# Attention, soft mixture of experts and a two-layer network on one core: ten ring slots, w_in and w_out loaded last, first token group in another order

## What is computed

```
attention:  q, k, v [4, 8, 576, 64]; scores = q k^T / 8 + bias by distance, causal window of 128, softmax, times v
x  = the heads side by side, 2304 tokens x 512
experts (soft mixture, 8 experts x 4 slots = 32 slots):
  logits = x @ phi;  d = softmax over tokens;  c = softmax over slots
  slot_input = d^T @ x                                   # 32 x 512
  slot_out[e] = relu(slot_input[e] @ w1[e]) @ w2[e]      # w1[e] 512 x 1024, w2[e] 1024 x 512
  y = c @ slot_out                                       # 2304 x 512
network:    h = relu(y @ w_in);  out = (h * h) @ w_out   # w_in 512 x 2048, w_out 2048 x 512
```

## Time and profile before

| | |
|---|---|
| median of three runs | 449.99 us (448.69 to 450.9) |
| the profiled execution | 451.01 us, span in the trace 449.4 us, mean granted clock of TensorE 0.973 |
| PE busy | 412.1 us, 92% of the span |
| DVE busy | 256.2 us, 57% |
| ACT busy | 208.4 us, 46% |
| last expert product ends | 215.40 us |
| first `project` starts | 230.86 us |
| share of PE in the chain that ended last | 78% |

### The profile page before, as it was taken

How to read it: one execution, slowest core, us unless ns; L and a number is a source line. 1 busy time by engine, 2 the same in 40 slices (tenths; PEclk the granted TensorE clock), 3 DMA queues, 4 the chain that set the end, 5 groups by cost and what they waited for, 6 DMA issues and landing times.

```text
span 449.4 us, 7858 instructions
## 1 busy us (share of the span) xinstructions
PE 412.1 (92%) x2851; PEld 312.3 (69%) x2851; DVE 256.2 (57%) x700; ACT 208.4 (46%) x541; POOL 71.7 (16%) x61
## 2 busy tenths in 40 slices
PE   4488999999989888966899999999999999999996
PEld 3376787878767544321368888888888888888884
DVE  3989989899872634210289745454444545454430
ACT  1456787877872311000197544434443444344420
POOL 2334556475660010000000000000000000000000
PEclk9979999999999989998599999999999999999999
DMA  5786999998743968999700100001010101010101
GB/s 135 170 233 177 231 265 237 255 259 202 188 112 131 402 254 300 413 388 387 291 0 1 47 2 16 30 1 47 2 47 2 47 0 47 0 47 0 48 0 47
DMA packets 73410, 61.35 MB, mean 137 GB/s; under 512 B 58784, under 2 KB 58784, under 8 KB 71328
## 3 DMA queue, kind: packets, MB, share of 16 engines
q1 hardware_dynamic: 73376, 60.89, 43.9%
HBM read 56.16 MB, written 4.72 MB: 135 GB/s over the span
## 4 chain that ended last, share of the span: by engine, by line
PE 78%; DVE 7%; ACT 5%; DMA 5%; SPq 3%; issue 1%; DVEq 0%
PE psum L1177 15%; PE psum L1175 15%; PE psum L1176 15%; ACT probs L752 4%; PE psum L943 4%; PE psum L961 4%; PE psum L1159 4%; PE psum L921 3%; DMA ring_late<-in_moe_w 3%; PE psum L1084 3%; PE psum L1105 2%; PE psum L892 2%; DMA q_in<-in_q 2%; PE psum L1013 2%; DVE rel_tail L497 1%; PE psum L905 1%
## 5 line engine op out<-in xcount | busy, mean ns | idle before, releaser
L1177 PE MATMUL psum<-wout_hi,act_lo 128*128 128x512 f32 x288 | 112.9, 392 | 0.0
L1175 PE MATMUL psum<-wout_hi,act_hi 128*128 128x512 f32 x288 | 112.9, 392 | 0.0
L1176 PE MATMUL psum<-wout_lo,act_hi 128*128 128x512 f32 x288 | 112.5, 391 | 0.0
L712 DVE TENSOR_TENSOR sq_h<-relu_h 128x512 f32<-128x512 f32 x72 | 49.8, 692 | 80.7 <-ACT relu_h L850 80.5
L850 ACT ACTIVATE relu_h<-psum 128x512 f32<-128x512 f32 x72 | 43.0, 598 | 91.6 <-PE psum L1159 87.7
L752 ACT ACTIVATE probs<-probs,row_min 128x256 f32<-128x256 f32 (+1 forms) x128 | 60.1, 471 | 37.4 <-DVE row_min L506 37.4
L460 POOL TENSOR_TENSOR probs<-probs,row_inv 128x1024 f32<-128x1024 f32 x31 | 59.2, 1930 | 57.2 <-DVE row_inv L555 57.2
L1177 PEld LDWEIGHTS psum<-wout_hi,act_lo 128*128 128x128 f32 x288 | 54.1, 188 | 11.7
L1176 PEld LDWEIGHTS psum<-wout_lo,act_hi 128*128 128x128 f32 x288 | 54.4, 189 | 8.9
L1175 PEld LDWEIGHTS psum<-wout_hi,act_hi 128*128 128x128 f32 x288 | 54.1, 188 | 9.0
L716 DVE TENSOR_TENSOR act_lo<-sq_h,act_hi 128x512 fp32r<-128x512 f32 x72 | 49.9, 693 | 5.4 <-ACT act_hi L853 0.7
(11 more groups left out here) (127 smaller groups left out, 424.7 us busy)
## 6 DMA issues: line engine op xcount, KB each, us to landing
ring<-in_moe_w SPq DMA_DIRECT2D x13, 1024.0 KB, 6.2
ring<-in_moe_w SPq DMA_DIRECT2D x5, 2048.0 KB, 15.8
ring_late<-in_moe_w SPq DMA_DIRECT2D x3, 2048.0 KB, 12.9
out_x<-out_sb SPq DMA_DIRECT2D x9, 512.0 KB, 2.8
q_in<-in_q SPq DMA_DIRECT2D x32, 128.0 KB, 5.6
k_in<-in_k SPq DMA_DIRECT2D x32, 128.0 KB, 3.0
v_in<-in_v SPq DMA_DIRECT2D x32, 128.0 KB, 3.1
win_sb<-in_moe_w_in SPq DMA_DIRECT2D x4, 1024.0 KB, 10.5
```

What stands on the lines that cost most here:

```text
L712: nc.vector.tensor_tensor(sq_h[:, u % 2, :], relu_h[:, u % 2, :], relu_h[:, u % 2, :], ALU.mult).then_inc(sq_done, 1)
L1175: mm(to, hi, wout_hi[:, c, :], start=first_of, stop=False)
L1176: mm(to, hi, wout_lo[:, c, :], start=False, stop=False)
L1177: last = mm(to, lo, wout_hi[:, c, :], start=False, stop=last_of)
```

## The change

Five things are done together.

1. `RING` is 10. Slots 8 and 9 are a new buffer `ring_x` that lies where `xT` was. SP loads item 8 there once 8 tiles of x are turned, item 9 after 16; item i goes to slot i mod 10. `LATE_ITEMS` has six items instead of eight, and `spare` now holds the first half of item 10.
2. w_in is no longer loaded at 146 us. Its place is taken by `ring_x`, so it comes after the last expert item and after `e2_done` 5, by column quarters of all rows (runs of 2 KB in memory instead of 8 KB), mixed with the quarters of w_out: w_in 0, 1, 2, w_out 0, w_in 3, w_out 1, 2, 3. `mix_parts(n)` waits for its own quarter only.
3. `wout_raw` moves from ring slots 0 and 1 to the place of `ring_late`, `mix` moves to that of `spare`.
4. The banks of `MIX_BANKS` change, so that from quarter 2 on the partial products use banks 6 and 7 and not those of the first output.
5. `first()` and `step(0)` of PE, ACT and DVE are written in another order: the sums and parts of quarters 2 and 3 stand between the first projects, and the splits of w_out stand behind them.

The core of the diff:

```diff
-RING, RW = 8, 4096
+RING, RW = 10, 4096
-LATE_ITEMS = (8, 10, 12, 9, 14, 11, 13, 15)
-SPLIT_ITEM = 8
+LATE_ITEMS = (10, 12, 11, 14, 13, 15)
+SPLIT_ITEM = 10
...
-            for i in range(EARLY, RING):
+            for i in range(EARLY, EARLY + 2):
                 load_item(sp, i)
-            for c in range(DC):
-                sp.wait_ge(xt_done, B * (c + 1))
-                sp.dma_start(win_sb[:, c, :], win_v[c]).then_inc(win_loaded[c], 16)
+            for i in range(EARLY + 2, RING):
+                sp.wait_ge(xt_done, 2 * B * (i - EARLY - 1))
+                load_item(sp, i)
             for i in LATE_ITEMS:
                 load_item(sp, i)
...
+            def load_win(n):
+                cols = slice(512 * n, 512 * n + 512)
+                sp.dma_start(win_sb[:, :, cols], win_v[:, :, cols]).then_inc(win_loaded[n], 16)
...
             sp.wait_ge(e2_done, 5)
+            load_win(0)
+            load_win(1)
+            load_win(2)
+            load_wout(0)
+            load_win(3)
+            load_wout(1)
...
DVE:
             def first():
+                take_mix(0)
+                take_part(1)
                 low_part(0, 0)
-                take_part(3)
-                take_mix(2)
                 low_part(1, 1)
-                split_low(1)
+                take_mix(1)
                 low_part(2, 2)
-                take_mix(3)
-                split_low(2)
                 low_part(3, 3)
-                split_low(3)
+                split_low(0)
...
+                    take_mix(2)
+                    split_low(1)
+                    low_part(4, 4)
+                    low_part(5, 5)
+                    take_part(3)
+                    split_low(2)
+                    take_mix(3)
+                    split_low(3)
+                    low_part(6, 6)
+                    low_part(7, 7)
+                    split_low(4)
+                    split_low(5)
...
PE:
             def first():
                 pe.wait_ge(combT_ready, QT)
                 mix_parts(0)
+                mix_sum(0)
                 mix_parts(1)
-                mix_sum(0)
+                pe.wait_ge(mix_ready, 1)
+                hidden(0, 0, 0)
+                hidden(0, 1, 1)
+                mix_sum(1)
                 mix_parts(2)
-                mix_sum(1)
...
+            def first_step():
+                project(0, 0, 0, 0)
+                mix_sum(2)
+                project(0, 1, 1, 0)
+                pe.wait_ge(mix_ready, 3)
+                hidden(0, 4, 4)
+                hidden(0, 5, 5)
+                mix_parts(3)
+                project(0, 2, 2, 0)
                 mix_sum(3)
+                project(0, 3, 3, 0)
+                pe.wait_ge(mix_ready, 4)
+                hidden(0, 6, 6)
+                hidden(0, 7, 7)
+                for u in range(AHEAD, FU):
+                    hidden(1, u + AHEAD, u + AHEAD - FU)
+                    project(0, u, u, 0)
```

More of the change, by code:

```diff
@@ L70, in attention_moe_ffn @@
     w2_v = w2.rearrange("e (a n) d -> e n a d", n=P)
[L71 removed]
+    win_v = w_in.rearrange("(p c) f -> p c f", c=DC)
     wout_v = w_out.rearrange("(a n) d -> n a d", n=P)
@@ L118, in attention_moe_ffn @@
         assert place["at"] == ring_end
+        spare_at = place["at"]
         spare = sb("spare", [P, RW // 2])
+        spare_end = place["at"]
+        place["at"] = spare_at
+        mix = sb("mix", [P, F2], F32R)
+        assert place["at"] <= spare_end
+        place["at"] = spare_end
         xT_at = place["at"]
@@ L125, in attention_moe_ffn @@
         xT_end = place["at"]
+        place["at"] = xT_at
+        ring_x = sb("ring_x", [P, 2, RW])
         place["at"] = xT_at
@@ L721, in first @@
             def first():
+                take_mix(0)
+                take_part(1)
                 low_part(0, 0)
-                take_part(3)
-                take_mix(2)
                 low_part(1, 1)
-                split_low(1)
+                take_mix(1)
                 low_part(2, 2)
-                take_mix(3)
-                split_low(2)
                 low_part(3, 3)
-                split_low(3)
+                split_low(0)
             def step(n, par):
[L734 to L737, removed]
+                if isinstance(n, int) and n == 0:
+                    take_mix(2)
[10 more added lines that the diff above has]
+                    split_low(5)
+                    split_low(6)
+                    split_low(7)
+                else:
+                    for u in range(AHEAD, FU):
+                        low_part(FU * n + u, u)
                 if not isinstance(n, int) or n < NFT - 1:
@@ L857, in first @@
             def first():
+                take_part(0)
+                take_mix(0)
                 high_part(0, 0)
                 high_part(1, 1)
-                take_mix(2)
-                split_high(2)
+                take_mix(1)
+                take_part(2)
                 high_part(2, 2)
-                take_mix(3)
                 high_part(3, 3)
-                split_high(3)
-                split_high(4)
+                split_high(0)
             def step(n, par):
[L869 to L872, removed]
+                if isinstance(n, int) and n == 0:
+                    take_mix(2)
+                    split_high(1)
+                    high_part(4, 4)
+                    high_part(5, 5)
+                    split_high(2)
+                    take_mix(3)
+                    split_high(3)
+                    high_part(6, 6)
+                    high_part(7, 7)
+                    split_high(4)
+                    split_high(5)
+                    split_high(6)
+                    split_high(7)
+                else:
+                    for u in range(AHEAD, FU):
+                        high_part(FU * n + u, u)
                 if not isinstance(n, int) or n < NFT - 1:
@@ L1135, in _ @@
             pe.wait_ge(soT_ready, 1)
-            for c in range(DC):
-                pe.wait_ge(win_loaded[c], 16)
             def mix_parts(n):
-                if n == 3:
-                    pe.wait_ge(mix_ready, 1)
+                pe.wait_ge(win_loaded[n], 16)
                 for c in range(DC):
```

46 lines of the change are left out of this document (18 added, 28 removed).

## The result

The changed kernel takes 466.94 us, the median of four runs (464.78 to 468.69), against 449.99 us before. The ratio is 1.0377, with a 95% interval from 1.0326 to 1.0427: 17 us slower. Forecast were 467.7 us in a range of 460 to 474. The profiled execution took 466.86 us, with a span of 465.2 us.

A forecast was written before the change was run, and what follows sets the result against it. Late expert items on full DMA engines, then a slow start of the network through ACT and DVE, were taken as the bound. Terms -7.4 + 18.8 + 6.3 = +17.7 us on 451.0 gave 468.7, median 467.7, range 460 to 474.

The forecast's parts named there:

- Part 1: End of the experts: with w_in loaded later, the last expert product ends at 204.3 us, a gain of 11.1 us.
- Part 2: Late w_in and w_out: each quarter lands before use (w_in 0 at 205.3 us), cost nothing, cover 2 to 8 us.
- Part 3: Way from the experts to the first project: project 0 starts at 223.5 us, 7.4 us earlier than before.
- Part 4: First projects: PE waits ahead of projects 1 to 4 (4.1, 6.0, 4.1, 5.5 us), making the stretch 18.8 us longer.
- Part 5: Clock around the first projects: PE's waits lower it, five slow stretches cost 6.3 us, bounds 0 and 11.1.
- clock stays up: Rival, first projects: everything as forecast but without the low clock's cost, 461.4 us; chance 0.15.
- clock stays down: Rival, projects 0 to 3 and the way to them: low clock throughout, 473.5 us; chance 0.10.
- Faster: Rival, first projects: waits stay under 7.4 us in sum and the early experts win, 444.6 us with all hidden; chance 0.05.
- Data late: Rival, last expert loads: the last half item lands 3 us later, everything shifts by 2.3 us, 470.0 us; chance 0.12.

The follow-up runs named there:

- the filled kernel: Changed kernel with 8, 20, 24, 20 and 12 products whose results are never read inside the waits ahead of projects 0 to 4: 466.31 us.
- the loads alone: Ring and loads of the changed kernel, with order and banks of the kernel before: 443.47 us, in the repeat 442.14.
- the order alone: Order and banks of the changed kernel, with ring and loads of the kernel before: 483.70 us, ratio to before 1.074.

## Why the prediction was right, step by step

- **Part 1** held. Forecast 204.3 us for the last expert product, measured 204.93; the first use of the first expert ended 0.8 us later in this execution (its release issued the load at 170.31 instead of 169.51 us), so at the same start it is within 0.2 us. No PE row of the last experts waits for a DMA. The cover is as thin as forecast: in the profiled execution of the filled kernel, with the same loads, PE waited 0.70 us for the last half item.
- **Part 2** held in its result. The landings were later than said: w_in 0 was issued at 196.38 and landed 11.3 us later, at 207.7, not 205.3, and PE took it at 208.21. The cover was 0.5 us, not 2.3. The forecast of 205.3 was the last half item at 202.6 plus 2.7 us for one unit. The half item was issued at 187.4 and landed 15.9 us later, at 203.3, 0.7 us late like the start; from it to w_in 0 it was 4.4 us and not 2.7, and from there on 2.7 for each quarter. Why the first quarter took 1.7 us more no run shows. The last quarter of w_out landed at 226.4 us, not 222.6; eight units of 2.7 us behind 202.6 would have given 224.2, so the prediction also slipped there. Nothing waited for either.
- **Part 3**: forecast 223.5, measured 224.43, of which 0.8 is the start. The low clock lay over part 0 and sum 0 (2.08 us for the sum instead of 1.13).
- **Part 4** decided. The rounds ahead of projects 1 to 4, from the end of one project to the start of the next, were 228.80 to 232.79 = 4.0 (forecast 4.1), 235.59 to 241.41 = 5.8 (6.0), 245.82 to 249.81 = 4.0 (4.1) and 252.66 to 257.84 = 5.2 (5.5). In sum 19.0 against 19.7. The runs that moved one split or one sum took out just the round that was named. One sign was stated wrongly: PE was to idle 3.5 to 5.5 us ahead of each of projects 1 to 4, and ahead of 1 and 3 it idled 2.97. The round of 4.1 us held the sum, 1.16 us in which PE works, so part 4's own terms give 3.0. Project 4 started at 257.84 us, 2 us ahead of the 260 forecast.
- **Part 5** was too high by 1.4 us. Projects 0, 2 and 4 ran at the low level for most of their length and cost 1.6, 1.6 and 1.6 us more (project 4 to 5 took 262.48 - 257.84 = 4.64 against 3.0), 4.9 in sum and not 6.3; I had counted five stretches. The rows of before could not give the number of such stretches: the run with the sum moved had the same waits less one and the low clock under all of its projects.

The Trainium skill ("TensorE: Matmul & The Clock Gate", section "Terms") would give half of the throttled time. The clocks of the four stretches after (0.71, 0.97, 0.86, 0.83) mean 5.8 + 0.6 + 2.8 + 3.4 = 12.6 us at the low level, so 6.3 us by the rule, against the 4.9 of the rows. The rule gives too much here; part of that time was wait, which no clock lengthens.
- **The sum**: -6.4 + (21.4 - 3.2) + 4.9 = +16.7, with the -0.8 behind project 8 15.9, against +17.7 forecast. (21.4 us is the growth from project 0 to 4; 3.2 of it is the low clock of projects 0 and 2, which the 4.9 hold.) The errors are +1.0 in part 3, -0.7 in part 4, -1.4 in part 5 and the -0.8 that no part had. Three point one way and one the other, and they leave the span 1.9 us under the forecast. That the medians lie only 0.8 us apart is luck: the forecast took off 1.0 us for the profiled execution of before, which lay above its median, and the profiled execution of the changed kernel lay at its own. The second series of the changed kernel had a median of 471.42 us, 3.7 above the forecast and still in its range.
- The rivals: "clock stays up" and "clock stays down" both fell with the stretches above, where the clock was at 0.71 to 0.97; with the sum moved it was at 0.66 to 0.68. "Faster" fell with the time itself. "Data late" was half right, since w_in 0 did land 2.4 us late, but PE waited for none of it.

## What to carry to other kernels

When a list of instructions is rewritten by hand, follow for each wait what stands ahead of the awaited instruction on its engine, and ahead of what that one awaits, until the chain ends or comes back to the engine it began on: one that comes back, as project - sum - rounding - split - project here, costs its whole length each time (4.0 us ahead of projects 1 and 3), however idle the engines are. Test a combined change in its parts; the loads alone were worth 6.3 to 8.3 us (449.76 - 443.47 and 450.45 - 442.14), and the order alone cost 28 us in its shortest execution (478.07 - 449.76) and 34 by the medians. And when a wait was taken out and the time doesn't move, read the granted clock of the stretch before giving up the theory.

## What the runs showed that was not expected

- The clock can hide a gain of 4 us in a kernel whose PE works in pieces. Filling the waits with useless products (64 of 0.12 us) made the kernel with the moved sum 9.4 us faster by the medians (468.02 to 458.65, timed on two chips whose medians for before are 449.64 and 450.45), of which the stretch from project 0 to 5 accounts for (262.68 - 223.96) - (256.47 - 225.60) = 7.9 us.
- Behind project 8 all kernels with the changed places of `mix` and `wout_raw` take 193.8 to 193.9 us, with either order, and those with the old places 194.6 us. A unit takes 2.98 instead of 2.99 us. Nothing in the rows says why.
- The executions differ by up to 5.7 us in when the experts end, in code that is alike: 204.2 to 209.9 us in the profiles with the changed loads. The clock has a part in it: from 170 to 200 us it was at 0.99 in the execution with 204.2, and at 0.92 and 0.90 in those with 209.5 and 209.9. The old order with the new loads shows the same behind the experts: they ended alike in its two profiles (204.62 and 204.67), but the clock from 215 to 225 us was 0.83 in one and 0.66 in the other, and project 0 started at 223.32 and 225.52.
- Two kernels (the changed one in its second series, the order alone) spread over 11 to 12 us, and in both the two longest executions have the lower mean clock. What brings the clock down in some executions and not in others is open, since only one execution of each series has a trace. The 5 us of the filled kernel are not explained by it: its longest execution has 0.969 and the others 0.972.
